# A three-layer attention and mixing kernel: channel chunks of 512 tokens, the accumulator's copy ahead of the exponent, and a first pair that loads one head twice

## What is computed

```python
def _attn_ref(q, k, v):
    q_pool = q.reshape(B, H, S // factor, factor, D).mean(axis=3)
    scores = scale * np.matmul(q_pool, k.transpose(0, 1, 3, 2))
    attn = np.exp(scores - np.max(scores, axis=-1, keepdims=True))
    return np.matmul(attn / (np.sum(attn, axis=-1, keepdims=True) + 1e-09), v)

def _moe_ref(x, w_in, g_ln, w_sg, b_sg, w_out):
    h = gelu_tanh(x @ w_in)                       # [4, 576, 1024]
    u, v = halves of h
    v_n = normalised v * g_ln
    v_s = np.einsum('ts,bsd->btd', w_sg, v_n) + b_sg[None, :, None]
    return x + (u * v_s) @ w_out

def _moe2_ref(x, w_tok1, w_tok2, w_ch1, w_ch2):
    xt = x.transpose(0, 2, 1)
    u = x + (np.maximum(xt @ w_tok1, 0.0) @ w_tok2).transpose(0, 2, 1)
    return u + np.maximum(u @ w_ch1, 0.0) @ w_ch2  # w_ch1 512x1536, w_ch2 1536x512
```

## Time and profile before

| | |
|---|---|
| median of 3 runs | 1067.08 us (1066.78 to 1069.34) |
| the profiled execution: its own time | 1067.29 us |
| its span | 1065.5 us |
| busy: PE, PEld | 1005.1, 870.1 us |
| busy: DVE, ACT, POOL | 595.9, 461.1, 378.1 us |

### The profile page before, as it was taken

How to read it: one execution, slowest core, us unless ns; L and a number is a source line. 1 busy time by engine, 2 the same in 40 slices (tenths; PEclk the granted TensorE clock), 3 DMA queues, 4 the chain that set the end, 5 groups by cost and what they waited for, 6 DMA issues and landing times.

```text
span 1065.5 us, 25232 instructions
## 1 busy us (share of the span) xinstructions
PE 1005.1 (94%) x9616; PEld 870.1 (82%) x9616; DVE 595.9 (56%) x1225; ACT 461.1 (43%) x898; POOL 378.1 (35%) x294
## 2 busy tenths in 40 slices
PE   3899999999999999879999999899999999999998
PEld 2666666666666666659999998888999999999998
DVE  3677777777777777669494948454322212212221
ACT  2677777777777777634151514152211201211210
POOL 3876666666666665531010103286000000000000
PEclk9999999999999999989999999999999999999999
DMA  6344443434344433310000000142000000000000
GB/s 221 91 113 112 111 111 111 111 111 111 111 111 111 111 86 104 119 36 1 1 0 0 0 1 23 30 129 79 1 23 0 22 22 0 22 22 0 22 22 22
DMA packets 34015, 64.80 MB, mean 61 GB/s; under 512 B 4160, under 2 KB 17088, under 8 KB 33984
## 3 DMA queue, kind: packets, MB, share of 16 engines
q1 hardware_dynamic: 33984, 64.37, 21.1%
HBM read 41.81 MB, written 4.72 MB: 44 GB/s over the span
## 4 chain that ended last, share of the span: by engine, by line
PE 66%; issue 21%; DVE 5%; ACT 3%; POOL 2%; DMA 1%; SPq 0%; ACTq 0%; DVEq 0%; POOLq 0%
PE ps L653 12%; PE ps L687 12%; PE ps L688 12%; PE ps L689 12%; PE ps L636 9%; PE ps L595 5%; DVE prob L1052 2%; ACT prob L876 2%; PE ps L624 1%; POOL rstd L557 1%; DVE pT L1067 1%; PE ps L625 1%; PE ps L626 1%; ACT xT L867 1%; DMA stage<-in_moe_w_in 1%
## 5 line engine op out<-in xcount | busy, mean ns | idle before, releaser
L1052 DVE TENSOR_SCALAR_CACHE_REDUCE prob<-ps 128x1152 f32<-128x1152 f32 x144 | 195.5, 1358 | 92.8 <-PE ps L636 72.7
L506 POOL TENSOR_SCALAR prob<-prob,rsum 128x1152 f32<-128x1152 f32 x144 | 176.8, 1228 | 136.5 <-DVE rsum L1061 136.0
L876 ACT ACTIVATE prob<-prob,nmax 128x1152 f32<-128x1152 f32 x144 | 181.4, 1259 | 21.3 <-DVE prob L1052 13.8
L653 PE MATMUL ps<-pT,v_sb 128*64 128x288 f32 x1152 | 170.6, 418 | 14.7 <-ACT xT L867 12.2
L867 ACT ACTIVATE pT<-ps 128x512 f32<-128x512 f32 (+1 forms) x288 | 110.2, 435 | 113.1 <-PE ps L595 112.6
L1015 ACT ACTIVATE f_h<-ps 128x288 fp32r<-128x288 f32 x96 | 39.4, 410 | 245.8 <-PE ps L689 245.8
L636 PE MATMUL ps<-k_over,q_over 64*128 64x288 f32 x768 | 138.2, 313 | 3.5 <-DVE prob L1052 3.5
L636 PEld LDWEIGHTS ps<-k_over,q_over 64*128 64x128 f32 x768 | 108.0, 189 | 23.8 <-DVE prob L1052 22.7
L653 PEld LDWEIGHTS ps<-pT,v_sb 128*64 128x64 f32 x1152 | 71.4, 136 | 56.3 <-issue 18.4
L595 PEld LDWEIGHTS ps<-ident,prob 64*128 64x128 f32 x2592 | 99.7, 140 | 19.7 <-issue 19.7
L687 PE MATMUL ps<-f_h,c_h 128*128 128x288 f32 x384 | 113.7, 296 | 0.0
(11 more groups left out here) (128 smaller groups left out, 2339.4 us busy)
## 6 DMA issues: line engine op xcount, KB each, us to landing
q_raw<-in_q SPq DMA_DIRECT2D x16, 640.0 KB, 4.2
k_raw<-in_k SPq DMA_DIRECT2D x16, 576.0 KB, 4.0
v_sb<-in_v SPq DMA_DIRECT2D x32, 288.0 KB, 2.9
k_over<-kh SPq DMA_DIRECT2D x32, 144.0 KB, 2.5
k_over<-kl SPq DMA_DIRECT2D x32, 144.0 KB, 2.6
out_x<-yT SPq DMA_DIRECT2D x8, 576.0 KB, 3.1
q_over<-qh SPq DMA_DIRECT2D x32, 128.0 KB, 2.2
q_over<-ql SPq DMA_DIRECT2D x32, 128.0 KB, 2.3
```

The lines of the kernel that those rows point to most:

```text
L506: g.tensor_scalar(sl, sl, rsum[:, s:s + 1], 0.0, ALU.mult, ALU.add).then_inc(norm_done, 1)
L653: ins = te.matmul(ps[PH * c:PH * c + PH, ACC_BANK, 0:n], v_sb[:, a, j, :], pT[:, a, j, c * n:c * n + n], start=(j == 0), stop=(j == KB - 1))
L876: sc.activation(sl, sl, ACT.Exp, scale=-1.0, bias=nmax[:, s:s + 1], accum_out=esum[:, s:s + 1]).then_inc(exp_done, 1)
L1052: ve.tensor_scalar(prob[:, PROB_BUF[s], :].rearrange("p (c n) -> p c n", c=SCORE_BANKS), ps[:, 0:SCORE_BANKS, 0:CK], -SCALE, BIG, ALU.mult ...
```

## The change

- **Channel stage.** Chunks of 512 tokens: the first 512 of each of the four batches, and a fifth chunk of the 4 x 64 tokens left. First and second product are interleaved: hidden tile f of the first product, then tile f - 2 of the second, into all four output tiles (one bank each). `f_h` and `f_l` are rings of four tiles. The sums go into `xT` in place; a batch is stored in one DMA, the left-over tokens in four.
- **ACT.** At steps 3 and 8 the copy of the accumulator stands ahead of the exponent.
- **First pair.** Head A's q and k are loaded twice, into both halves of the partitions, ahead of all other loads (k from ACT's queue, q from SP's) and split apart: k in two pieces, each waited for by half of the first scores. Only head B is put over. The full q and k follow; POOL splits that k, DVE that q between its first reads of scores. POOL's work for the next pair begins three steps later.
- **PE** transposes the identity 52 times at the start, and 36 times (64 wide) ahead of the scores in each of the first four steps.
- **POOL's weight pieces** are split in high and low halves with other work between, in the last three pairs.

```diff
@@ PE, start and scores
+                if isinstance(i, int) and i + a == 0:
+                    cols = slice(c * CK, (c + 1) * CK)
+                    return (qh_two[half, q0:q0 + P], ql_two[half, q0:q0 + P], kh_two[half, cols], kl_two[half, cols])
...
+                    if s == 0 and zero:
+                        pe.wait_ge(two_split, 2 + m)
...
+                if first and s < LAG:
+                    for n in range(2 * KB):
+                        for h in range(2):
+                            half = slice(h * PH, h * PH + PH)
+                            te.transpose(ps[:, TRANS_BANK + h, n % 8 * PH:(n % 8 + 1) * PH], ident[half, :], ident[half, half])
...
+            with pe.Fori(0, 13):
+                for n in range(4):
+                    te.transpose(ps[:, TRANS_BANK, n * P:(n + 1) * P], ident[:, :], ident[:, :])
@@ SP, start
+            for half in range(2):
+                sp.dma_start(q_two[half * PH:(half + 1) * PH, :, :], q[0, 0:PH, :, 0:4 * P]).then_inc(q_two_in, 16)
+            sp.wait_ge(q_two_in, 32)
+            sp.wait_ge(k_two_in, 32)
+            load_k(0)
             load_q(0)
-            load_k(0)
             sp.wait_ge(q_summed, 1)
             load_q(1)
+            sp.wait_ge(k_split, 1)
+            load_k(1)
             sp.wait_ge(q_split, 1)
-            sp.wait_ge(k_split, 1)
-            put_over(0, 0)
             put_over(1, 0)
-            load_k(1)
@@ ACT, step of the attention
+                if not first and s in (TAIL_STEP - 1, NS - 1):
+                    acc_copy(i - 1, 0 if s == TAIL_STEP - 1 else 1)
                 if s >= 1 and not tail:
                     exps(i, s - 1)
                 elif s == 0 and not first:
                     exps(i - 1, NS - 1)
-                if not first and s in (TAIL_STEP - 1, NS - 1):
-                    acc_copy(i - 1, 0 if s == TAIL_STEP - 1 else 1)
@@ POOL
+            body(NP - 3, 1, w0=0, w=(7, 8))
+            body(NP - 2, 0, w0=1, w=(7, 8))
+            body(NP - 1, 1, last=True, w0=2, w=(0, 2, 4, 6))
@@ PE, channel stage
             def chunk(c):
...
+                for f in range(CHT + F_LAG):
+                    if f < CHT:
+                        first_product(c, f)
+                    if f >= F_LAG:
+                        second_product(c, f - F_LAG)
+
+            with pe.Fori(0, B) as c:
                 chunk(c)
+            chunk(B)
@@ SP, stores
+                sp.wait_ge(y_free, at(b, KT_N, Y_N + KT_N))
+                sp.dma_start(out_v[:, bass.ds(b * KT_N, KT_N), 0:CN], xT[:, bass.ds(b * KT_N, KT_N), 0:CN]).then_inc(stored, 16)
+            for e in range(KT_N):
+                sp.wait_ge(y_free, Y_N + KT_N * B + e + 1)
+                sp.dma_start(out_v[:, e:NP:KT_N, CN:SQ], xT[:, e:NP:KT_N, CN:SQ]).then_inc(stored, 16)
```

More of the change, by code:

```diff
@@ L92, in tile_of @@
         return s if s < TAIL_STEP else s - TAIL_STEP - 1
+    F_N, F_LAG = 4, 2
+    CN = 4 * P
+    LEFT = SQ - CN
     top = ExitStack()
@@ L858, in _, with first_product @@
-            with pe.Fori(0, 2 * B) as c:
+            def first_product(c, f):
+                pe.wait_ge(f_free, at(c, CHT, f + 1))
+                n = B * LEFT if isinstance(c, int) and c == B else CN
+                sl = slice(f * P, (f + 1) * P)
+                for kt in range(KT_N):
+                    if f == 0:
+                        pe.wait_ge(u_split, at(c, KT_N, kt + 1))
+                    ins = three(ps[:, f % F_N, 0:n], c1_h[:, kt, sl], c1_l[:, kt, sl],
+                                u_h[:, kt, 0:n], u_l[:, kt, 0:n], kt == 0, kt == KT_N - 1)
+                ins.then_inc(f_mm, 1)
@@ new lines, in second_product @@
+            def second_product(c, f):
+                pe.wait_ge(f_free, at(c, CHT, F_N + f + 1))
+                n = B * LEFT if isinstance(c, int) and c == B else CN
+                for e in range(KT_N):
+                    if f == 0:
+                        pe.wait_ge(y_free, at(c, KT_N, e + 1))
+                    sl = slice(e * P, (e + 1) * P)
+                    ins = three(ps[:, 4 + e, 0:n], c2_h[:, f, sl], c2_l[:, f, sl],
+                                f_h[:, f % F_N, 0:n], f_l[:, f % F_N, 0:n], f == 0, f == CHT - 1)
+                    if f == CHT - 1:
+                        ins.then_inc(y_mm, 1)
@@ L867, in copy @@
                 return sc.activation(o, i_, ACT.Copy)
-            act.wait_ge(k_in, 16)
-            copy(kh2[:, 0, :], k_raw[:, :]).then_inc(k_high, 1)
+            for half in range(2):
+                act.dma_start(k_two[half * PH:(half + 1) * PH, :], k[0, 0:PH, :]).then_inc(k_two_in, 16)
+            act.wait_ge(k_two_in, 32)
+            for m in range(2):
+                cols = slice(m * 2 * CK, (m + 1) * 2 * CK)
+                copy(kh_two[:, cols], k_two[:, cols]).then_inc(k_two_high, 1)
             def exps(i, s):
@@ L1006, in _, with u_hi_of, chunk @@
             act.wait_ge(u_added, ONE + KT_N)
[L1008 removed]
+            def u_hi_of(c):
                 for e in range(KT_N):
[L1010 to L1012 removed]
+                    copy(wide(c, u_h[:, e, :]), slab_of(c, e)).then_inc(u_hi, 1)
+            def chunk(c):
+                n = B * LEFT if isinstance(c, int) and c == B else CN
                 for f in range(CHT):
[L1014 to L1025 removed]
+                    act.wait_ge(f_mm, at(c, CHT, f + 1))
+                    sc.activation(f_h[:, f % F_N, 0:n], ps[:, f % F_N, 0:n], ACT.Relu).then_inc(f_hi, 1)
+            u_hi_of(0)
+            with act.Fori(0, B - 1) as c:
+                chunk(c)
+                u_hi_of(c + 1)
+            chunk(B - 1)
+            act.wait_ge(u_added, ONE + KT_N * B)
+            u_hi_of(B)
+            chunk(B)
         @block.vector
@@ L1087, in step @@
                     take(i, s)
+                    if first:
+                        first_q(s)
             for s in range(NS):
```

200 lines of the change are left out of this document (102 added, 98 removed).

## The result

| | us |
|---|---|
| kernel before, 4 runs | 1066.93 median (1065.16 to 1069.34) |
| changed kernel, 4 runs | 1042.96 median (1041.75 to 1043.86) |
| ratio | 0.9773, 95% interval 0.9751 to 0.9795 |
| profiled execution, changed | 1043.86 (span 1042.0) |
| forecast, range | 1038.7, 1035.5 to 1047.5 |

The change takes off 24.0 us, 2.3%. The forecast was 28.6. The time lies in the range, 4.3 us above the forecast, and that remainder is what the experiments look for.

A forecast was written before the change was run, and what follows sets the result against it. The prediction took PE, busy 94% of the span, to bound the kernel. Terms 11.0 - 0.2 + 12.2 - 1.8 + 7.4 = 28.6 us, taken from 1067.3, gave 1038.7 us, range 1035.5 to 1047.5.

The forecast's parts named there:

- Channel chunks: Channel stage: 1440 matmuls for 2304, same columns, 296.2 us instead of 307.2, a gain of 11.0 us.
- Rival B: Channel stage: a 512-column matmul takes the gated row's 0.2330 us, 6.8 us less gain, 1045.5 us; chance 0.24.
- rival E: Channel stage: denser work is granted less clock; slower below a mean grant of 0.91, about 1072 at 0.90; chance 0.04.
- The 0.2 us at the first chunk: First channel chunk: wider split delays DVE's token-mix sums by about 1 us, of which 0.2 us reaches PE.
- The end: After the last matmul: four stores instead of one last store, gain 0, from -1 to +1 us.
- Accumulator copy: Pair boundaries: ACT's copy ahead of the exponent removes PE's 15 waits, a gain of all 12.2 us.
- rival D: Pair boundaries: another engine's next wait takes the place, half of the 12.2 us stays, 1045 us; chance 0.07.
- POOL's splits: Last three pairs: weight splits make PE wait 0.7 and 2.5 us, a 1.4 us wait goes; net -1.8 us.
- The 0.7 of pair NP-2: After weight split 0 on POOL: PE's transposes three steps on wait about 0.7 us.
- The head: Start and first pairs: 6.7 us gained, 0.9 lost on pair 1's copies, 1.6 gained; net 7.4 us.
- steps of 2.61: Head: after a first score at 11.0 us, score steps take 2.61 us instead of 3.30.
- Rival C: Head: transposes do not raise the clock, first score at 15.1 us, 8.4 us less gain, 1047 us; chance 0.15.

The follow-up runs named there:

- e2: Changed kernel with POOL's first subtraction (low part of k) held until DVE has summed the raw q; 1039.72 us.
- e4: Changed kernel without the 52 transposes of the identity and without the small ones of the first four steps; 1042.39 us.
- e1: Changed kernel with the first half of weight split 2 on POOL moved one step later in the last pair; 1038.93 us.
- e3: Changed kernel with POOL splitting the weights wo only after DVE's last low part of x, at the gated stage's start; 1036.11 us.
- e6: Changed kernel with the channel stage of before put back (eight chunks of 288 columns, 2304 matmuls); 1053.05 us.
- e7: Changed kernel with the edits of e1 and e2, the wait of e3, and the first two weight splits one step earlier; 1033.55 us.
- e9: e7 without the small transposes (36 in each of the first four steps), the 52 wide ones kept; 1037.72 us.
- e5: Changed kernel with ACT's copy of the accumulator put back behind the exponent; 1049.77 us.
- e8: e7 with 24 transposes of the identity added in PE's idle time before the gated stage; 1034.24 us.
- e10: Kernel before, with POOL splitting the weights wo only after DVE's last low part of x; 1062.69 us.

## Why the prediction came out as it did

- **Channel chunks, +11.0: right.** 295.7 us for 296.2, steps of 0.2267 for 0.2271. The fixed 13.3 ns of a matmul holds at 256, 288 and 512 columns. Rival B (0.2330) falls, rival E too (granted 1.00). The 0.2 us at the first chunk did not occur: the last token-mixing matmul stands at 742.44, the first channel matmul at 742.57. The end gave 0.6 (3.87 us behind the last matmul, 4.47 before), inside the ±1.
- **Accumulator copy, +12.2: right in mechanism, a little high.** Twelve boundaries gave 9.2, 0.77 each, where 12.2/15 is 0.81; the period is 25.89 and 26.04 in turn, forecast 25.8. Some of it went to the next in line, as rival D has it: PE's wait on DVE before tail scores is 4.5 us for 3.4, of which 0.5 is pair 0's. The last of the fifteen gave 0.2: the 0.75 us on ACT's copy at 444.69 is gone, but PE waits 0.40 at 436.66 for DVE's copy of a transposed tile.
- **POOL's splits, -1.8: the place right, the size wrong.** The 0.7 of pair NP-2 came (the boundary's gain is cancelled there). The wait in the last pair was forecast at 2.5 and is 3.0. The step that failed is the next: I counted a wait as its length. It was followed by 6.8 us at half clock. The two intervals lost 3.35 us: 0.8 and 1.4 gained as forecast, 3.0 lost in the wait and 2.5 more with the half clock. With the split moved the last two come off, 5.4 us. The strip of the earlier trace rows could have warned me: its one low slice stands where PE idles, at the gated stage's start.
- **The head, +7.4: 4.0 short.** The first score at 11.3 for 11.0, short matmuls: right. The step of the forecast that failed is "steps of 2.61". I let DVE's sum of the raw q lie beside POOL's subtraction of k as if neither touched the other; the sum took 2.4 us more, and PE waited 2.45. The e2 run has the steps I forecast (10.87, 13.68, 16.23, 19.12, tail 21.76; forecast 11.0, tail 21.4) and its first mark at 47.52 is 5.7 better than before. The other 1.7 to 7.4: the step after the tail stands at 25.5 for 24.8, having waited 1.24 us for the copies of head B that I called just in time, and pair 1 waits 1.76 for its copies, not 0.9. In the changed kernel's profiled run about 1.4 went to half clock between 34 and 41 on top. So the 4.0 are about 0.9 for the standstill, as far as it reaches the first mark (47.52 against the mean of 48.17 and 48.60), 1.4 for the clock and 1.7 for the copies. No run takes the double load of head A back by itself; its worth is read from the marks alone.
- **Rival C: wrong.** The clock rises under transposes alone, at about 7.3 us (forecast 6.4), and their price was right (0.214 and 0.109 us, forecast 0.22 and 0.11). What I took for the worth of that rise, 8.4 us, was too much: without all transposes (e4) the first mark comes 2.3 us later, and still 2.6 us before that of the kernel before. Rival C's sum was off by itself: -1.7 - 0.4 + 1.6 - 0.9 is -1.4, not about -1. And it kept the 52 slow transposes in front of the first score, which e4 leaves out, so e4 is not rival C's case to the letter.
- **Luck:** 1.9 us in the gated stage, since the changed kernel's profiled run lacks the stretch at half clock that the kernel before has at 676 to 680. Eight of the twelve profiled kernels have it (before, e1, e2, e3, e4, e6, e7, e9), four don't (after, e5, e8, e10). It is no effect of the change. Without it the profiled run would have stood at 1045.8: in the range still, but nearer to the times of rivals B and D than to the forecast.

Open: what decides whether a stretch at half clock comes in a given run, and its length (3.4 to 13.6 us here). That these stretches make the 1 to 5 us of spread between runs of one kernel is argued, not shown, since only one run of each has a trace.

## What to carry to other kernels

Where PE is never idle, the number of matmuls has a price of its own: widen the moving operand until a bank is full, and take the step from a row of the same kind. Before an operation is called hidden on DVE or POOL, look whether both then read SBUF, and two operands at once above all; a wait that makes one go after the other can be worth more than the overlap, if the collision does not just move to the next operation. A wait of 2 to 3 us on PE can cost more than its length, because a stretch at half clock may follow, and on an in-order engine nothing that waits for a DMA should stand ahead of a result that PE wants.

## What the runs showed of the hardware

- The matmuls of the channel stage cost columns/2.4 GHz + 13.3 ns: 0.1200 us (256), 0.1333 (288), 0.2267 (512). In the gated stage, where the table streams, one of 512 took 0.2330; why is not known.
- DVE's operations with two operands from SBUF stand still beside POOL's subtractions: 640 columns in 3.26 us beside POOL, 0.82 alone; four of 576 columns in 8.09 and 2.77. A conversion took 1.45 and 0.48. DVE's read of PSUM is untouched (1.36 both ways).
- Transposes raise the granted clock and keep it: thin ones of 64 rows by 64 columns between the score groups kept it at 2.4 GHz where 1.5 us of idle time in each step otherwise brought 13.6 us at 1.2 GHz (e7 and e9, 2.8 us at the first mark).
- After PE waits of 2.1 to 3.0 us in the last pair the grant fell to 0.50 for 3.4 to 6.8 us in four profiled runs of five, and in none of the seven with a shorter wait there. In the head the same is less regular: behind PE's wait of 2.2 to 2.5 us before the third score group, with small transposes after it, the grant fell in e1 and e3 (for 3.4 us from 19.0 and 19.2) and not in the changed kernel and e6.
